# Scores of the first 64 tokens with the first 64 keys alone, in an fp32 mLSTM and two gated feed-forward layers

## The reference

```python
m_new = max(f[t] + m, i[t]);  f_stab = exp(f[t] + m - m_new);  i_stab = exp(i[t] - m_new)
C = f_stab * C + i_stab * outer(v[t], k[t]);   n = f_stab * n + i_stab * k[t]
y[t] = sigmoid(o[t]) * (C @ q[t]) / max(abs(n @ q[t]), 1)
```

## Time and profile before

| | |
|---|---|
| median of 3 runs | 450.05 us (450.0 to 450.38) |
| the profiled execution | 450.07 us |
| its span, first to last instruction | 448.2 us |
| around the span | 1.87 us |
| TensorE busy | 444.2 us, 99% |
| VectorE, ScalarE, GpSimd busy | 215.6, 183.7, 87.2 us |
| granted TensorE clock | 1.00 |

### The profile page before, as it was taken

How to read it: one execution, slowest core, us unless ns; L and a number is a source line. 1 busy time by engine, 2 the same in 40 slices (tenths; PEclk the granted TensorE clock), 3 DMA queues, 4 the chain that set the end, 5 groups by cost and what they waited for, 6 DMA issues and landing times.

```text
span 448.2 us, 10567 instructions
## 1 busy us (share of the span) xinstructions
PE 444.2 (99%) x4494; PEld 405.5 (90%) x4494; DVE 215.6 (48%) x475; ACT 183.7 (41%) x358; POOL 87.2 (19%) x131
## 2 busy tenths in 40 slices
PE   9999999999999999999999999999999999999997
PEld 5899999999999999988889988889988899888897
DVE  6876927854556456424432227560055630256510
ACT  7885377534753473214543154331033320223310
POOL 3567710112010200004656181000000000000000
PEclk9999999999999999999999999999999999999999
DMA  8975600221122114000433010000000000000000
GB/s 235 308 257 144 163 3 3 82 82 38 48 80 69 37 31 153 8 2 20 142 106 117 17 44 1 1 1 29 31 2 0 1 16 29 16 2 1 1 29 29
DMA packets 10430, 26.69 MB, mean 60 GB/s; under 512 B 1504, under 2 KB 4608, under 8 KB 10384
## 3 DMA queue, kind: packets, MB, share of 16 engines
q1 hardware_dynamic: 10128, 25.96, 18.9%
q10 hardware_dynamic: 256, 0.07, 0.1%
HBM read 23.97 MB, written 1.97 MB: 58 GB/s over the span
## 4 chain that ended last, share of the span: by engine, by line
PE 99%; ACT 0%; issue 0%; DVE 0%
PE bank L1218 37%; PE bank L1169 21%; PE bank L1237 10%; PE bank L1238 9%; PE bank L1239 9%; PE bank L1076 3%; PE bank L1107 3%; PE bank L1010 2%; PE bank L1249 1%; PE bank L1095 1%; PE bank L1046 1%; PE bank L1116 1%; PE bank L1264 0%; PE bank L1256 0%; PE bank L1272 0%; PE bank L1060 0%
## 5 line engine op out<-in xcount | busy, mean ns | idle before, releaser
L1218 PE MATMUL bank<-x_hi,wgv_hi 64*128 64x512 f32 x576 | 105.8, 388 | 0.0
L689 ACT ACTIVATE sg<-bank 128x256 f32<-128x256 f32 (+1 forms) x96 | 47.1, 492 | 131.2 <-PE bank L1218 82.5
L1218 PE MATMUL bank<-x_lo,wgv_hi 64*128 64x512 f32 x480 | 93.8, 386 | 0.0
L960 DVE TENSOR_TENSOR bank<-sg,bank 128x256 f32<-128x256 f32 (+1 forms) x96 | 53.8, 560 | 58.0 <-ACT sg L689 56.5
L1169 PE MATMUL bank<-x_hi,wgv_hi 128*128 128x256 f32 x288 | 80.4, 290 | 0.0
L1169 PE MATMUL bank<-x_lo,wgv_hi 128*128 128x256 f32 x288 | 77.7, 282 | 0.0
L1237 PE MATMUL bank<-wo_hi,h_hi 128*128 128x320 f32 x240 | 75.4, 314 | 0.0
L1218 PE MATMUL bank<-x_hi,wgv_lo 64*128 64x512 f32 x384 | 75.1, 386 | 0.0
L1239 PE MATMUL bank<-wo_hi,h_lo 128*128 128x320 f32 x240 | 74.1, 309 | 0.0
L1238 PE MATMUL bank<-wo_lo,h_hi 128*128 128x320 f32 x240 | 74.1, 309 | 0.0
L1218 PEld LDWEIGHTS bank<-x_hi,wgv_hi 64*128 64x128 f32 x576 | 54.4, 184 | 11.5 <-issue 0.7
(11 more groups left out here) (143 smaller groups left out, 538.7 us busy)
## 6 DMA issues: line engine op xcount, KB each, us to landing
step<-in_qk_t SPq DMA_DIRECT2D x24, 192.0 KB, 3.8
step<-in_vok SPq DMA_DIRECT2D x12, 324.0 KB, 3.2
step<-in_w_gv SPq DMA_DIRECT2D x6, 576.0 KB, 3.6
raw_x<-in_w_gv SPq DMA_DIRECT2D x4, 576.0 KB, 7.9
raw_p<-in_w_gv SPq DMA_DIRECT2D x4, 576.0 KB, 5.8
step<-in_vok SPq DMA_DIRECT2D x10, 160.0 KB, 5.8
raw_p<-in_w_o SPq DMA_DIRECT2D x3, 480.0 KB, 3.3
y<-y_tok SPq DMA_DIRECT2D x9, 160.0 KB, 1.8
```

What stands on the lines that cost most here:

```text
L689: act.activation(sg_view(n), g_view(n), ACT.Sigmoid).then_inc(sg_done, 1)
L960: dve.tensor_tensor(v_view(n), sg_view(n), v_view(n), ALU.mult).then_inc(hf_done, 1)
L1218: mm = pe.matmul(ps(n), w, x, start=own and (s, p) == (0, 0), stop=last and not own)
```

## The change

It touches tiles 2 to 11. For these tiles the even heads of S stay as they were for the first 64 keys, and their last 64 keys are taken against the last 64 tokens alone. For the odd heads, the first 64 keys against the first 64 tokens go to the upper half of the output, the first 64 keys against the last 64 tokens to the lower half, and the last 64 keys against the last 64 tokens to the upper. So in the columns of the first 64 tokens one half of the partitions holds the first 64 keys and the other half nothing new: the upper for even heads, the lower for odd ones. d_lhs is written to match: in the columns of the first 64 tokens both halves stand for the first 64 keys (`keys`), and the mask repeats.

In N the first 64 tokens take their values from two new small arrays, one for even and one for odd heads, in which the other half's 64 rows are zero (`va0`, zeroed once by GpSimd, filled by two more transfers per tile from a new input `v_first`). The matmuls still run over 128 rows. TensorE waits for these transfers and for the zeros.

```diff
@@ load_vo @@
+                if n >= B:
+                    sp.dma_start(va0[b][0][0:HALF, :], v_first[n, 0, :, :]).then_inc(v0_in[b], 16)
+                    sp.dma_start(va0[b][1][HALF:P, :], v_first[n, 1, :, :]).then_inc(v0_in[b], 16)
@@ GpSimd @@
-            hide_of(0, 2)
+            pool.tensor_copy(d_lhs[HALF:P, 0, :, :], hide[HALF:P, :, :]).then_inc(hide_done, 1)
+            hide_of(1, 2)
+            for b in range(B):
+                pool.memset(va0[b][0][HALF:P, :], 0.0).then_inc(zeros_done, 1)
+                pool.memset(va0[b][1][0:HALF, :], 0.0).then_inc(zeros_done, 1)
@@ rows, parts 1 to 3, sub 2 and sub 3 @@
-                    high = dve.tensor_copy(d_lhs[0:R, j0:j1, :, :], halves(i_r[:, cs]))
+                    for w in range(2):
+                        high = dve.tensor_copy(lhs(0, j0, j1, w), keys(i_r[:, cs], w))
-                    dve.tensor_tensor(d_lhs[Q:Q + R, j0:j1, :, :], halves(i_r[:, cs]),
-                                      d_lhs[0:R, j0:j1, :, :].bitcast(F32), ALU.subtract).then_inc(lhs_done, 1)
+                    for w in range(2):
+                        low = dve.tensor_tensor(lhs(Q, j0, j1, w), keys(i_r[:, cs], w),
+                                                lhs(0, j0, j1, w).bitcast(F32), ALU.subtract)
+                    low.then_inc(lhs_done, 1)
@@ S, tiles 2 to 11 @@
+                    lower, upper = slice(0, HALF), slice(HALF, P)
+                    for c in range(0, HG, 2):
+                        for h, half, ks, ts in ((c, lower, lower, slice(0, P)), (c, upper, upper, upper),
+                                                (c + 1, upper, lower, lower), (c + 1, lower, lower, upper),
+                                                (c + 1, upper, upper, upper)):
                             for i in range(2):
                                 rs = slice(HALF * i, HALF * i + D)
-                                mm = pe.matmul(score_bank(n, i)[us, c * P:(c + 1) * P], sq[b][rs, 1, c, us],
-                                               sq[b][rs, 0, c, :], start=True, stop=True)
+                                mm = pe.matmul(score_bank(n, i)[half, h * P + ts.start:h * P + ts.stop], sq[b][rs, 1, h, ks],
+                                               sq[b][rs, 0, h, ts], start=True, stop=True)
@@ N @@
+                    if n >= B:
+                        pe.wait_ge(v0_in[b], 32 * j)
+                        pe.wait_ge(zeros_done, 4)
...
+                            values = [va[b][:, h * D1:(h + 1) * D1]] * 2
+                            if n >= B:
+                                values[0] = va0[b][h % 2][:, h // 2 * D1:(h // 2 + 1) * D1]
                             for u in range(2):
                                 us = slice(HALF * u, HALF * u + HALF)
                                 mm = pe.matmul(bank[base(n) + 2][us, h * D1:(h + 1) * D1], wexp[b][:, h, us],
-                                               va[b][:, h * D1:(h + 1) * D1], start=True, stop=True)
+                                               values[u], start=True, stop=True)
```

More of the change, by code:

```diff
@@ L76, with mlstm_moe_kernel @@
 SPLIT_AT = {0: [4], 2: [5], 3: [6], 4: [7], 5: [8], 7: [9], 8: [10], 9: [11]}
-def mlstm_moe_kernel(nc, gates, qk_t, vok, w_gv, w_o, rms_g, out):
+def mlstm_moe_kernel(nc, gates, qk_t, vok, v_first, w_gv, w_o, rms_g, out):
     ctx = ExitStack()
@@ L163, in mlstm_moe_kernel @@
         kn = [t[:, QK + HE + DM:QK + VOK] for t in step]
+        va0 = [(tails[b][:, H * P + HE:H * P + HE + KV], step[b][:, QK + VOK:QK + VOK + KV]) for b in range(B)]
         raw0 = [t[:, :] for t in (raw_p, raw_q, raw_x2, raw_x3, raw_x0, raw_x1)]
@@ L292, in mlstm_moe_kernel @@
         vo_in = [sem(f"vo_in{b}") for b in range(B)]
+        v0_in = [sem(f"v0_in{b}") for b in range(B)]
+        zeros_done = sem("zeros_done")
         kn_in = [sem(f"kn_in{b}") for b in range(B)]
@@ L533, in piece @@
                     pool.tensor_tensor(cst[b][:, :], cst[b][:, :], cnew[:, :], ALU.add).then_inc(cst_done, 1)
+            for b in range(B):
+                pool.memset(va0[b][0][HALF:P, :], 0.0).then_inc(zeros_done, 1)
+                pool.wait_ge(zeros_done, 2 * b + 1)
+                pool.memset(va0[b][1][0:HALF, :], 0.0).then_inc(zeros_done, 1)
+                pool.wait_ge(zeros_done, 2 * b + 2)
             pool.memset(eps[:, :], EPS).then_inc(consts, 1)
@@ L757, in link, with twice, keys, lhs @@
                 dve.wait_ge(dve_link, links[0])
-            def halves(row):
+            def twice(row):
                 return row.rearrange("r (j t) -> r j t", t=P).unsqueeze(2).to_broadcast([R, row.shape[1] // P, 2, P])
+            def keys(row, w):
+                r = row.rearrange("r (j u t) -> r j u t", u=2, t=HALF)
+                return r if w else r[:, :, 0, :].unsqueeze(2).to_broadcast([R, row.shape[1] // P, 2, HALF])
+            def lhs(p0, j0, j1, w):
+                return d_lhs[p0:p0 + R, j0:j1, :, w * HALF:w * HALF + HALF]
             def rows(part, sub):
@@ L1028, in piece @@
                 if kind == "D":
-                    pe.wait_ge(hide_done, 1 if j == 1 else 2)
+                    pe.wait_ge(hide_done, 3 if j == 1 else 5)
                     pe.wait_ge(lhs_done, part_of(j))
@@ L1070, in piece @@
                         pe.wait_ge(p_done, 2 * n)
-                    for c in range(HG):
-                        for u in range(2):
-                            us = slice(HALF * u, HALF * u + HALF)
+                    if n < B:
+                        for c in range(HG):
+                            for u in range(2):
+                                us = slice(HALF * u, HALF * u + HALF)
+                                for i in range(2):
+                                    rs = slice(HALF * i, HALF * i + D)
+                                    mm = pe.matmul(score_bank(n, i)[us, c * P:(c + 1) * P], sq[b][rs, 1, c, us],
+                                                   sq[b][rs, 0, c, :], start=True, stop=True)
+                                    if c == HG - 1 and u == 1:
+                                        mm.then_inc(s_done, 1)
+                        return
+                    lower, upper = slice(0, HALF), slice(HALF, P)
[3 more added lines that the diff above has]
+                                                (c + 1, upper, upper, upper)):
                             for i in range(2):
                                 rs = slice(HALF * i, HALF * i + D)
-                                mm = pe.matmul(score_bank(n, i)[us, c * P:(c + 1) * P], sq[b][rs, 1, c, us],
-                                               sq[b][rs, 0, c, :], start=True, stop=True)
-                                if c == HG - 1 and u == 1:
+                                mm = pe.matmul(score_bank(n, i)[half, h * P + ts.start:h * P + ts.stop], sq[b][rs, 1, h, ks],
+                                               sq[b][rs, 0, h, ts], start=True, stop=True)
+                                if h == HG - 1 and ks == upper:
                                     mm.then_inc(s_done, 1)
@@ L1307, in _ @@
                         piece(("O", NT - B + t))
-_INS = ["gates", "qk_t", "vok", "w_gv", "w_o", "rms_g"]
+_INS = ["gates", "qk_t", "vok", "v_first", "w_gv", "w_o", "rms_g"]
 def kernel(q, k, v, i_gate, f_gate, o_gate, moe_w_gate, moe_w_val, moe_w_out,
```

18 lines of the change are left out of this document (13 added, 5 removed).

## The result

The changed kernel takes **448.59 us** (448.05 to 448.97, median of 7 runs), the kernel before in the same rounds 450.05 us (449.82 to 450.47). The ratio is 0.9965, with a 95% interval of 0.9955 to 0.9974: faster by 0.35%. The profiled execution took 448.17 us with a span of 446.3 us, at a granted clock of 1.000.

What follows compares the result with a forecast made beforehand. TensorE, busy 444.2 of 448.2 us, was taken to bound the kernel. From 450.07 us, -1.76 + 0.11 + 0.05 = -1.60 gave 448.47; with the runs' median of 450.05, 448.5 us was forecast, range 448.0 to 450.2.

Steps and rivals of the forecast that it cites:

- TensorE's saving, 1.76 us: Scores of tiles 2 to 11: the busier, upper quarter takes 0.696 us for 0.872, saving 0.176 a tile.
- VectorE, 0.16 us later and 0.11 for TensorE: Start, near 21 us: split gate-row copies and subtractions delay weight chunk 1; TensorE waits 0.11 us (0 to 0.25).
- The 0.05 deducted near 52 us: Last out-weight chunk on GpSimd: TensorE, arriving 0.24 us earlier, may meet it; 0.05 us of gain deducted by estimate.
- GpSimd at its own work, transfers, waits, 0: GpSimd's extra copies and memsets, 20 more SyncE transfers and TensorE's added waits are all hidden: cost 0.
- Sum: Against the profiled execution of 450.07 us: -1.76 + 0.11 + 0.05 = -1.60 us.
- at 0.053 a pass: Scores, with the skill page's 53 ns weight load for 64 columns as pass cost: saving 2.4 us in place of 1.76.
- Order binds: Scores: a matmul may not end before the one issued ahead; 0.80 us a tile, 449.45 us in all; chance 13%.
- Same quarter twice costs: Scores: successive matmuls on the upper quarter each show 0.05 us; 0.125 more a tile, 451.4 us; chance 10%.
- Columns aren't the cost: Scores: moving columns aren't what a pass costs; 0.0715 us a pass, 450.0 us results; chance 8%.
- More is lost at the start: Start: VectorE and DMA upper ends together, 0.25 and some 0.5 us, leave 449.1 us; chance 9%.

Runs made afterwards that it cites:

- the even-form kernel: Changed kernel with the odd heads scored in the even heads' form, 16 matmuls a tile in place of 20: 450.05 us, ratio 0.9996 to the kernel before.
- the half-columns kernel: Changed kernel with its 64-column score matmuls cut to 32 moving columns: 448.6 us, ratio 0.9962 to the kernel before.
- all upper ones first: Changed kernel with the same twenty score matmuls a tile, all upper-quarter ones issued ahead of the lower: 453.18 us, ratio 1.0073 to the kernel before.

## Why the prediction was right

It said 448.5 us; 448.59 was measured. The mechanism that carries the number held; the terms around it did less well. Step by step:

- **TensorE's saving, 1.76 us: the mechanism held, 1.61 measured.** The busier quarter sets the cost (the even-form kernel), and a pass with 64 weight columns costs nearly the same at 32 and at 64 moving columns (the half-columns kernel), 0.058 us in the trace with all upper ones first. Read to where all quarters meet again, a tile saves 0.16 to 0.17 us for the 0.176 worked out: the state's part starts 0.20 earlier, but staggered, and takes 0.03 to 0.04 more.
- **VectorE, 0.16 us later and 0.11 for TensorE: right in place, too small.** The run became 4.20 - 3.91 = 0.29 us longer and TensorE lost 0.26, beyond the upper end of 0.25. The way from one engine to the other was right (21.00 to 21.11). What was missing is GpSimd. The prices for halves and wholes were those of an idle GpSimd: there they nearly hold, with 0.06 and 0.07 us more for two halves in part 3 (0.48 for 0.42 and 0.75 for 0.68; for part 1 it was priced at 0.08 each). In part 1, GpSimd's subtraction lies beside the second half copy, and the two copies take 0.64 where I had 0.35; before, it lay beside the subtraction, which took 0.57 where I had 0.41, and whose halves took 0.48 where I had 0.49. In all nine traces with divided rows the second half copy ends 0.07 to 0.09 us behind GpSimd's instruction. That it waits for GpSimd is the reading that fits; no run here moves that instruction away, so it is not shown by experiment.
- **The 0.05 deducted near 52 us: nothing there.** In the changed kernel's trace TensorE does not wait at 52 us. With the gap at 21 us removed a wait of 0.16 us appears, and the even-form kernel's trace has both.
- **GpSimd at its own work, transfers, waits, 0: no cost seen**, by the kernel without the transfers, zeros and waits.
- **Sum.** -1.61 + 0.26 = -1.35 by the traces, -1.46 by the medians, against -1.60 predicted. The saving was put 0.15 too high and the start's loss 0.15 too low, both to the fast side; the 0.05 deducted went against them. That 448.5 lies within 0.1 us of the median is in part luck, as executions differ by more than that (448.05 to 448.97).

One figure beside the sum was wrong: at 0.053 a pass the lower quarter would bind with 4 x (0.109 + 0.053) = 0.648, so the saving would be 2.2 us and not 2.4.

The rivals. *Order binds* fell in the form given, 0.80 us a tile. What I cited for it, the Trainium skill, "TensorE: Matmul & The Clock Gate", section "What overlaps and what doesn't", has matmuls start and end in program order, and for the starts the trace disagrees: with all upper matmuls first, lower ones start between 36.02 and 36.03 when 18 of the 24 upper passes issued ahead of them have started. The ends are modelled in the profile, so it says nothing of them. But the rival had a real core. The changed kernel's order never asks TensorE to look past more than one waiting matmul for each half of rows; two other orders of the same work do, and are slower than the kernel before. *Same quarter twice costs*: refuted, a tile became 0.16 to 0.17 us shorter where it had 0.125 longer. *Columns aren't the cost*: it had 0.0715 a pass and nothing gained; refuted by 0.058 a pass and by the half-columns kernel. *More is lost at the start*: the loss exists, 0.26 us and not 0.75.

## What to carry to other kernels

Price packed small matmuls by quarter of the array: list what each quarter gets, take the pass cost of each shape, and the busiest list is the time; 25% fewer columns were worth nothing until they were spread. Then issue the quarters alternately: in the orders tried here a bad one cost 3.7 to 4.6 us. Measure a piece to where all quarters meet again, not to the first start of the next piece. Before you price a short VectorE instruction, look at what GpSimd does beside it. And where several engines pace each other at the start, take a gap away in an experiment before counting it as gain, and compare traces whose transfers landed alike.

## What was not expected of the hardware

- The limited look-ahead past a busy quarter: 0.03 to 0.08 us a tile where at most one waiting matmul has to be passed, 0.38 and 0.49 where it is three and more, with the same twenty matmuls.
- VectorE subtractions of 16x128 with both inputs on chip took 0.48 us for two, and 1.59 us beside GpSimd's subtractions of 128x256. A copy of 16x128 took 0.20 us, and 0.51 beside GpSimd's subtraction of 64x128.
